# Splitting w_in by halves, with the low part of its u half summed by a transfer, and normalising v on ScalarE

## What is computed

```python
h = x @ w_in                       # x: 768 x 384 per batch, w_in: 384 x 1024
h = gelu_tanh(h)
u, v = h[..., :512], h[..., 512:]
mu = mean(v, -1); var = mean((v - mu) ** 2, -1)
v_n = (v - mu) / sqrt(var + 1e-06) * g_ln
v_s = einsum('ts,bsd->btd', w_sg, v_n) + b_sg[None, :, None]
x = x + (u * v_s) @ w_out
```

## Time and profile before

| | before |
|---|---|
| median of 3 runs | 724.77 us |
| profiled execution | 725.26 us |
| its span | 723.5 us |
| granted clock of TensorE, mean | 0.995 |
| TensorE busy | 707.4 us (98%) |
| VectorE busy | 453.7 us (63%) |
| ScalarE busy | 198.3 us (27%) |
| GpSimd busy | 77.5 us (11%) |
| chain that ended last | TensorE 84%, VectorE 10%, issue 2% |

### The profile page before, as it was taken

The page is one execution under the profiler, slowest core; times in us unless marked ns, Lnnn a source line. Parts: engine busy times, 40 slices in busy tenths (PEclk is TensorE's granted clock), DMA queues, the critical chain, the costliest instruction groups (busy, mean ns, idle before and its releaser), DMA issues.

```text
span 723.5 us, 13389 instructions
## 1 busy us (share of the span) xinstructions
PE 707.4 (98%) x5538; PEld 679.3 (94%) x5538; DVE 453.7 (63%) x869; ACT 198.3 (27%) x369; POOL 77.5 (11%) x125
## 2 busy tenths in 40 slices
PE   7799989999999999999999999999999999999998
PEld 6688989889998999989999999999999999999998
DVE  7997868897778967668686746373543726331212
ACT  1438111342114421144316221232122321122111
POOL 1023000030001200051111321002200100000000
PEclk9999999999999999999999999999999999999999
DMA  9757232331322122071325412002210200000000
GB/s 285 214 138 180 56 95 84 88 94 51 100 83 83 51 76 73 35 243 44 110 77 183 125 44 68 1 34 66 80 31 11 77 10 33 0 34 1 0 33 34
DMA packets 21438, 56.50 MB, mean 78 GB/s; under 512 B 2404, under 2 KB 14824, under 8 KB 21384
## 3 DMA queue, kind: packets, MB, share of 16 engines
q1 hardware_dynamic: 18104, 44.53, 20.3%
q0 software_dynamic: 3136, 11.07, 5.8%
q10 hardware_dynamic: 144, 0.13, 0.1%
HBM read 46.26 MB, written 9.46 MB: 77 GB/s over the span
## 4 chain that ended last, share of the span: by engine, by line
PE 84%; DVE 10%; issue 2%; POOL 1%; ACT 1%; DMA 1%; SPq 0%; DVEq 0%; POOLq 0%
PE bank L1166 74%; PE bank L1197 3%; PE bank L1229 2%; PE bank L1224 1%; PE bank L1385 1%; PE bank L1214 1%; DVE fwd L916 1%; DVE rev L904 1%; PE bank L1187 1%; PE bank L1261 1%; DVE u_kept L1126 1%; DMA decay_k_q<-in_akq 1%; DVE sm L934 1%; DVE state_decayed L928 1%; POOL x_quarters L649 1%
## 5 line engine op out<-in xcount | busy, mean ns | idle before, releaser
L1166 PE MATMUL bank<-ut_hi,w_c 128*128 128x384 f32 x576 | 162.8, 339 | 0.0
L1113 DVE SCALAR_TENSOR_TENSOR hidden_lo<-bank,hidden_hi 128x384 fp32r<-128x384 f32 x96 | 53.3, 555 | 124.8 <-ACT hidden_hi L838 123.5
L1166 PEld LDWEIGHTS bank<-ut_hi,w_c 128*128 128x128 f32 x576 | 105.4, 188 | 0.0
L838 ACT ACTIVATE hidden_hi<-bank 128x384 fp32r<-128x384 f32 x96 | 47.3, 492 | 196.9 <-PE bank L1166 196.9
L1166 PE MATMUL bank<-w_c_hi,hidden_hi 128*128 128x384 f32 x288 | 96.6, 336 | 0.5 <-DVE u_kept L1126 0.5
L1166 PE MATMUL bank<-w_c_hi,hidden_lo 128*128 128x384 f32 x288 | 96.3, 334 | 0.0
L1166 PE MATMUL bank<-ut_lo,w_c 128*128 128x384 f32 x288 | 96.3, 334 | 0.0
L1166 PE MATMUL bank<-w_c_lo,hidden_hi 128*128 128x384 f32 x288 | 96.2, 334 | 0.0
L1166 PE MATMUL bank<-w_sg_hi,vn_hi 128*128 128x384 f32 x192 | 67.1, 349 | 0.3 <-issue 0.3
L1166 PE MATMUL bank<-w_sg_lo,vn_hi 128*128 128x384 f32 x192 | 64.8, 337 | 0.0
L1166 PE MATMUL bank<-w_sg_hi,vn_lo 128*128 128x384 f32 x192 | 64.7, 337 | 0.0
(11 more groups left out here) (193 smaller groups left out, 1389.8 us busy)
## 6 DMA issues: line engine op xcount, KB each, us to landing
decay_k_q<-in_akq SPq DMA_DIRECT2D x19, 673.8 KB, 5.1
x_scratch<-x_half SPq DMA_DIRECT2D x8, 579.0 KB, 4.2
out_tiles<-u_kept SPq DMA_DIRECT2D x24, 192.0 KB, 2.0
values<-in_v SPq DMA_DIRECT2D x18, 192.0 KB, 5.1
x_quarters<-x_scratch SPq DMA_DIRECT2D x16, 168.9 KB, 3.9
raw_first_a<-in_w_first SPq DMA_DIRECT2D x3, 768.0 KB, 10.9
raw_first_b<-in_w_first SPq DMA_DIRECT2D x3, 768.0 KB, 7.5
raw_weights_b<-in_w_second SPq DMA_DIRECT2D x3, 768.0 KB, 4.3
```

Source lines behind the costliest of these rows:

```text
L838: nc.scalar.activation(hid[0][:, i % 4, :], HB[i % 2][:, 0:HS], ACT.Relu).then_inc(hhi_done, 1)
L1113: nc.vector.scalar_tensor_tensor(out=hid[1][:, i % 4, :], in0=HB[i % 2][:, 0:HS], scalar=0.0, in1=f32(hid[0][:, i % 4, :]), op0=ALU.max, o ...
L1166: ins = nc.tensor.matmul(dst, a, c, start=start and n == 0, stop=stop and n == len(passes) - 1)
```

## The change

It has two parts.

**w_in by halves.** The host lays w_in out as the 512 v columns (all three k) and then the 512 u columns, so piece 0 is the v half and piece 1 the u half. Piece 1 joins SUMMED: VectorE's second split of w_in goes, ScalarE gets a negation between the second w_in_hi and x_hi of tile 0, and GpSimd an accumulating transfer ahead of that of piece 2. A v product of batch 0 waits for the low part of piece 0 alone, a u product for the transfer. SyncE's load of piece 3, into piece 1's buffer, waits for the high part of piece 1 and no longer for its low part.

**The normalisation of v.** `v_norm` moves from VectorE to ScalarE, as Identity(v * rs + sh) in place, with sh = -mean * rs. GpSimd computes nm = -mean and sh = nm * rs besides ve and rs. On ScalarE v_norm(i - 1) comes between gelu(i) and vn_hi(i - 2), and the last one in u 1 (in "v end" 0 for batch 0). There is no other table load.

```diff
-             + [("query", 3), ("carry", 2), ("scores", 2), ("split", 0), ("out", 2), ("x", 0), ("split", 1)]
+             + [("query", 3), ("carry", 2), ("scores", 2), ("split", 0), ("out", 2), ("x", 0)]
...
-             + [("split", 0), ("split", 1), ("x", 0), ("out", 2), ("x", 1), ("split", 2), ("neg", 2), ("x", 2)]
+             + [("split", 0), ("split", 1), ("neg", 1), ("x", 0), ("out", 2), ("x", 1), ("split", 2), ("neg", 2), ("x", 2)]
...
-FIRST_POOL = [("sum", 2), ("v", 0), ("v", 1), ("v", 2), ("sum", 3), ("v", 3), ("sum", 4), ("v", 4), ("v", 5)]
+FIRST_POOL = [("sum", 1), ("sum", 2), ("v", 0), ("v", 1), ("v", 2), ("sum", 3), ("v", 3), ("sum", 4), ("v", 4), ("v", 5)]
...
-SUMMED = (2, 3, 4)
+SUMMED = (1, 2, 3, 4)
...
-        w_in = [place(f"w_in_{x}", [P, KD, FF], F32R, at_w + i * 4 * KD * FF) for i, x in enumerate(("hi", "lo"))]
+        w_in = [place(f"w_in_{x}", [P, 2 * KD, FV], F32R, at_w + i * 4 * KD * FF) for i, x in enumerate(("hi", "lo"))]
...
                                         ALU.add).then_inc(ve1_done, 1)
+                nc.gpsimd.tensor_tensor(nm1[:, t % 3:t % 3 + 1], mv1[:, t % 3, 0:1], mone[:],
+                                        ALU.mult).then_inc(nm1_done, 1)
                 pool.wait_ge(ve1_done, i + 1)
                 nc.gpsimd.tensor_tensor(rs1[:, t % 3:t % 3 + 1], ve1[:, t % 3:t % 3 + 1], mhalf[:, 0:1],
                                         ALU.pow).then_inc(rs1_done, 1)
+                pool.wait_ge(rs1_done, i + 1)
+                pool.wait_ge(nm1_done, i + 1)
+                nc.gpsimd.tensor_tensor(sh1[:, t % 3:t % 3 + 1], nm1[:, t % 3:t % 3 + 1], rs1[:, t % 3:t % 3 + 1],
+                                        ALU.mult).then_inc(sh1_done, 1)
...
+            def v_norm(b, t):
+                act.wait_ge(sh1_done, NT * b + t + 1)
+                nc.scalar.activation(vg[:, t % 3, :], vg[:, t % 3, :], ACT.Identity, scale=rs1[:, t % 3:t % 3 + 1],
+                                     bias=sh1[:, t % 3:t % 3 + 1]).then_inc(vnorm_done, 1)
...
                     nc.scalar.activation(vg[:, i % 3, :], v_bank(b, i)[:, 0:FV],
                                          ACT.Gelu_apprx_tanh).then_inc(vg_done, 1)
+                    if i >= 1:
+                        v_norm(b, i - 1)
                     if i >= 2:
                         vn_hi(b, i - 2)
...
                         gate(b, i)
+                        if i == 1:
+                            v_norm(b, NT - 1)
                         if i in (2, 3):
                             vn_hi(b, NT - 4 + i)
...
                 elif step == "v end":
+                    if c == 0:
+                        v_norm(0, NT - 1)
                     vn_hi(0, NT - 2 + c)
...
-            def v_norm(b, t):
-                i = NT * b + t
-                dve.wait_ge(rs1_done, i + 1)
-                nc.vector.tensor_scalar(vg[:, t % 3, :], vg[:, t % 3, :], mv1[:, t % 3, 0:1], rs1[:, t % 3:t % 3 + 1],
-                                        ALU.subtract, ALU.mult).then_inc(vnorm_done, 1)
...
                     nc.vector.bn_aggr(mv1[:, i % 3, :], stats1[:, i % 3, :]).then_inc(mv1_done, 1)
-                    if i >= 1:
-                        v_norm(b, i - 1)
...
-                        wait_lo(pe, 1)
+                        wait_lo(pe, 0)
...
-                            [([x[:, k, i * P:(i + 1) * P] for x in xs], [w[:, k, FV:FF] for w in w_in])
+                            [([x[:, k, i * P:(i + 1) * P] for x in xs], [w[:, k, :] for w in w_in])
...
-                        [([w[:, k, f * P:(f + 1) * P] for w in w_in],
+                        [([w[:, KD + k, f * P:(f + 1) * P] for w in w_in],
...
-        "w_first": np.concatenate([by_rows(inputs["moe_w_in"]), by_rows(inputs["moe_w_out"]),
+        "w_first": np.concatenate([by_rows(inputs["moe_w_in"][:, FV:]), by_rows(inputs["moe_w_in"][:, :FV]),
+                                   by_rows(inputs["moe_w_out"]),
                                    by_rows(inputs["moe_w_sg"].T)], 1),
```

More of the change, by code:

```diff
@@ L199, in build @@
         ve1 = place("ve1", [P, 3], F32, region(12))
+        nm1 = place("nm1", [P, 3], F32, region(12))
+        sh1 = place("sh1", [P, 3], F32, region(12))
+        mone = place("minus_one", [P, 1], F32, region(4))
         stats2 = place("stats2", [P, NT, 6], F32, region(144))
@@ L362, in build @@
         rs1_done = sem("rs1_done")
+        nm1_done = sem("nm1_done")
+        sh1_done = sem("sh1_done")
         vnorm_done = sem("vnorm_done")
@@ L614, in _ @@
             nc.gpsimd.memset(eps_c[:], EPS)
+            nc.gpsimd.memset(mone[:], -1.0)
             nc.gpsimd.memset(mhalf[:], -0.5).then_inc(memset_done, 1)
@@ L1002, in phase1 @@
                     elif step == "u":
-                        if i == 0:
-                            v_norm(b, NT - 1)
                         if i in (2, 3):
@@ L1146, in _ @@
                 elif step == "v end":
-                    if c == 0:
-                        v_norm(0, NT - 1)
                     v_lo(0, NT - 2 + c)
```

## The result

The changed kernel takes 743.76 us (median of 4 runs, 742.85 to 745.7); the kernel before, run beside it, 724.85 (723.93 to 725.44). The ratio is 1.0257, 95% interval 1.0238 to 1.0276: 18.9 us slower, 5.6 more than forecast (738.2). The median lies inside the range by 0.24 us of its end of 744, and two of the four runs (744.62, 745.7) lie beyond it. One execution of the kernel before, run beside e8, e10 and e11, took 3512.67 us and counts in none of the ratios. The profiled span is 741.0 us against 723.5.

The account below looks back on a forecast made before the run. VectorE was taken to set the pace in batch 0's first stage, with later TensorE waits lost for good. Terms -1.4 + 8.1 + 5.2 + 1.5 = +13.4 took the median from 724.77 to 738.2 us, range 728 to 744.

Parts of the forecast that it names:

- First v product near 30.5: Batch 0, TensorE: the first v product, held until 31.57 before, would start at about 30.5 us.
- Landing of the new transfer: Batch 0: the low u half lands 8.0 to 10.4 us after issue; the first u product waits 0 to 0.5.
- Rival (c): Batch 0: the low u half's transfer takes over 14 us, adding 3 us to the forecast, 741; chance 0.08.
- The lower bound of -2.8: Batch 0: w_in by halves, valued at -1.4 us, reaches -2.8 if the clock also does not fall at 32 us.
- Batch 0 of part 2: Batch 0: ScalarE's queue with the normalisation only eats part of w_in by halves' gain, counted in the -1.4 us.
- Last batch, +8.1: Last batch: the last vn_lo ends 8.1 us late and the z step moves from 339.84 to 347.9; bounds 5 and 10.
- Turn of vn_lo 4.1: Last batch, v steps: vn_lo start to start takes 4.1 us and not 2.63, 1.5 more in each of three turns.
- Batches 1 and 2, +2.6 each: Batches 1 and 2: late vn_lo, qu, kn and masked scores cost 2.6 us each, 5.2 together; bounds 1.2 and 3.5 each.
- Clock, +1.5 with bounds 0 to 3: Last batch: TensorE idles about 3.3 us before z, and the lower clock costs 1.5 us; bounds 0 and 3.
- Rival (a): Batches 1 and 2 cost nothing as VectorE catches up, the last batch as forecast: 733.0 us; chance 0.15.
- (b): V steps: GpSimd's scalars always come before ScalarE reaches v_norm, only batch 0's gain remains: 722 to 723.5 us; chance 0.10.
- (d): Whole kernel: the two effects cancel to within 1.5 us if TensorE has more cover than seen: 725 us; chance 0.05.

Follow-up runs that it names:

- e8: Kernel before, with 6 matmuls that nothing reads in TensorE's wait for qu of chunk 3 of batch 1; 723.96 us, ratio 0.9977.
- e10: e1 with the first u product moved on TensorE behind tile 3's transposes and chunk 4's attention output, its gelu on ScalarE moved too; 725.93 us, ratio 0.9997.
- e11: e10 with the filling matmuls of e8 added; 724.17 us, ratio 0.9978.
- e4: e1, but the load of piece 3 goes out only when the accumulating transfer into the low u half has landed; 729.76 us, ratio 1.0066.
- e1: Kernel before with w_in by halves alone, the normalisation staying on VectorE; 727.56 us, ratio 1.0035.
- e3: Kernel before with the layout and waits of w_in by halves, the low u half still made by VectorE, no added transfer; ratio 1.0007.
- e2: Kernel before with the normalisation moved to ScalarE alone, w_in split as before; 744.04 us, ratio 1.0245.
- e5: e2, but on ScalarE the pass for tile i-2 stands behind gelu(i), directly ahead of its vn_hi; 731.12 us, ratio 1.0084.
- e7: e2, but in the last batch VectorE normalises as before and GpSimd makes no nm and sh; 735.0 us, ratio 1.0119.

## Why the prediction was right, and where it was wrong

The sign, the mechanism of part 2 and the larger terms were right. That the range held was luck in part: batch 0 was wrong by 5.8 us, and the median stayed inside by 0.24. By its steps:

- **First v product near 30.5:** 30.12.
- **Landing of the new transfer (8.0 to 10.4 us, so a wait of 0 to 0.5, "hidden"):** wrong, and the step that turned -1.4 into a loss. 11.9 us, a wait of 3.29. I had bounded it by the rows of three other transfers, though I had written that piece 3's load would go out beside it; without that load it took 10.1 (e4). Rival (c) was this mechanism. TensorE reached the product at 37.43, 8.7 us behind the issue at 28.7, so each us above 8.7 and not above 14 is a wait, and the product stands first in TensorE's queue (e10). e1: +2.2 us in place of -1.4. The 1.66 us of VectorE did appear, 1.7 at 37 us, and were gone behind this wait. The lower bound of -2.8 had no ground: e3 had the higher clock at 32 us and won nothing.
- **Batch 0 of part 2 ("only eats part of the gain"):** wrong, 4.3 us (e2). ScalarE waits there for sh too, 5.1 us in two waits of e2 between 40 and 80 us, and with the pass one place later (e5), where neither wait is there, batch 0 costs 1.7. TensorE being late already was no cover; VectorE, which sets the pace there, waits for ScalarE's gelu and vn_hi by 8.5 us between 40 and 80 us in e2 and by 3.4 before.
- **Last batch, +8.1:** 7.5; with the old order there it is nothing (e7). Turn of vn_lo 4.1: 4.09, with a wait for sh of 1.35 in each. TensorE waits 3.1 us for fold_lo and 0.3 for vn_lo, and 3.2 more for the gelus of the u and v steps, 6.6 in all where I wrote about 6 for the first two. Two durations inside were off and cancel: the pass is 0.81 us long and 0.72 from start to start, not 0.62 and 0.51, and GpSimd's chain takes 1.10 to 1.2 and not 1.4, since nm and sh did not add 0.26 each: ve, nm and rs start 0.14 apart. That an operation is long beside the fold was right: 1.63, and 3.44 of waiting behind it.
- **Batches 1 and 2, +2.6 each:** 2.1 in each in the changed kernel, 2.4 and 2.3 in e2. TensorE waits for qu (1.4 us in four) and sm (2.0 in two) as named, and not for kn.
- **Clock, +1.5 with bounds 0 to 3:** 2.9 in this execution, 1.5 in e2's and 1.6 in e5's. The place was right, and the size is not fixed. My trace of before held one such loss at 104 us that need not be there in other executions; the changed kernel's did not have it, so the clock came to a net 1.4 by luck.
- **Rival (a), batches 1 and 2 free:** no. **(b), scalars in time:** no, but e5 shows the order in which they are, 13 us better. **(d):** no.

Sum: +3.2 at 139 us (4.4 of batch 0, less the 1.5 of clock at 104 us, and 0.3 of small steps), 4.2, 7.5 and 2.9, together 17.8; at the end of the span it is 17.5, where 13.4 was forecast. By terms the difference of 4.1 is 5.8 of batch 0, less 1.0 and 0.6 by which the other batches fell short, and -0.1 of clock (1.4 against 1.5) and small steps. The medians differ by 18.9 and not 17.5, as the profiled execution of the changed kernel lies 0.9 under its median and that of the kernel before 0.4 over its own.

## What to carry to other kernels

An operation moved to a less busy engine is priced by what it waits for at its new place in that engine's order, and by who stands behind it; let it stand where its inputs are a turn old. A transfer put in place of an engine's work is priced with the loads of that very stretch beside it, and the product that needs it goes behind other work. Before an in-order queue is held back, read what stands behind the held entry.

## What was not expected of the hardware

- An accumulating transfer of 768 KB took 6.8 us (e2, w_sg_lo) to 12.2 us (e10, w_in_lo). The mean DMA share was 0.90 over the slow one and 1.00 over one of 7.3 us in e2, so the share alone does not tell the time. The Trainium skill ("DMA: Bandwidth & Descriptors", anatomy of a GpSimd-issued DMA) has a fit for DMAs issued by GpSimd, without a word on accumulating ones, from which one estimates 3.8 us for 768 KB; no accumulating transfer here comes near it.
- ScalarE's pass over 128x512 with a scale and a shift for each partition took 0.81 us, the plain conversion of the same tile 0.61.
- A GpSimd operation on 128x1 took 0.19 us (the power rs 0.55), or 1.63 (ve, changed kernel) to 2.23 (ve, e5) with VectorE's fold of 1.75 us beside it: whichever of ve, nm and rs came there was the long one. The Trainium skill ("GPSIMD Engine Reference", Specifications) says that GpSimd shares its SBUF interfaces with VectorE and contends with VectorE instructions that have two SBUF inputs, as the fold has; the runs agree.
- The clock fell, or not, behind a wait of 1.4 to 1.7 us at the same place in executions of nearly the same program, and cost 0, 1.5 or 3 us there; with the wait filled it did not fall in the profile (e8).
